# Attention and two feed-forward layers on one core: loads cut to the rows with data, a spread by ScalarE, all block inverses on GpSimd, other PSUM banks in the prologue

## The reference

```python
for t in range(S):
    y[:, :, t] = einsum('bhd,bhde->bhe', rt, state)
    Sa = einsum('bhde,bhe->bhd', state, at)
    state = state * wt[:, :, None, :] - einsum('bhd,bhe->bhde', Sa, bt) + einsum('bhd,bhe->bhde', vt, kt)
h = x @ w_in;   solu = h * softmax(h);   x = (layernorm(solu) * g_ln) @ w_out
h = x @ w2_in;  x = (max(h, 0) + alpha * min(h, 0)) @ w2_out
```

## Time and profile before

| | before |
|---|---|
| median of 3 runs | 1088.87 us |
| profiled execution, its own time | 1090.63 us |
| its span | 1088.6 us |
| mean granted clock of TensorE | 0.945 of full |
| busy: PE, DVE, ACT, POOL | 955.0, 642.5, 406.1, 224.3 us |
| last store of attention issued | at about 489 us |

### The profile page before, as it was taken

How to read it: one execution, slowest core, us unless ns; L and a number is a source line. 1 busy time by engine, 2 the same in 40 slices (tenths; PEclk the granted TensorE clock), 3 DMA queues, 4 the chain that set the end, 5 groups by cost and what they waited for, 6 DMA issues and landing times.

```text
span 1088.6 us, 32820 instructions
## 1 busy us (share of the span) xinstructions
PE 955.0 (88%) x14112; PEld 903.2 (83%) x14112; DVE 642.5 (59%) x1120; ACT 406.1 (37%) x842; POOL 224.3 (21%) x442
## 2 busy tenths in 40 slices
PE   3377889788978888885899999999999999999998
PEld 2366778677867877874899999999999999999987
DVE  6864666475756764357465564746546474664644
ACT  2112333242423342325444353534435363443533
POOL 4362463355336434200000000000000000000000
PEclk9588999898999999896999999999999999999999
DMA  7527455655665564316200000000000000000000
GB/s 259 103 78 187 119 153 132 169 139 166 167 142 161 158 170 102 90 43 182 62 2 25 11 15 25 2 24 0 24 12 12 24 0 24 0 24 12 2 13 13
DMA packets 145925, 82.91 MB, mean 76 GB/s; under 512 B 119824, under 2 KB 129168, under 8 KB 145808
## 3 DMA queue, kind: packets, MB, share of 16 engines
q1 hardware_dynamic: 145808, 81.17, 27.4%
HBM read 61.49 MB, written 19.66 MB: 75 GB/s over the span
## 4 chain that ended last, share of the span: by engine, by line
PE 61%; issue 14%; POOL 10%; DVE 6%; SPq 6%; DMA 2%; ACT 1%; DVEq 0%; ACTq 0%; POOLq 0%
PE acc L916 6%; PE acc L918 5%; PE acc L917 5%; PE bank L916 5%; PE bank L918 5%; PE bank L917 5%; POOL s_x L695 4%; PE mid L916 4%; PE mid L918 4%; PE mid L917 4%; POOL s_t L693 4%; SPq L202 4%; PE px L292 2%; PE mid L969 2%; PE mid L970 2%
## 5 line engine op out<-in xcount | busy, mean ns | idle before, releaser
L1250 DVE SCALAR_TENSOR_TENSOR stage<-mid,slope 128x512 f32<-128x512 f32 x96 | 66.4, 692 | 110.0 <-ACT slope L1092 110.0
L1146 POOL TENSOR_TENSOR stats<-stats,consts 128x1 f32<-128x1 f32 x24 | 13.2, 549 | 571.5 <-DVE stats L1228 571.5
L916 PE MATMUL acc<-wo_h,act_h 128*128 128x320 f32 x384 | 122.5, 319 | 7.2 <-DVE act_l L1160 6.4
L918 PE MATMUL acc<-wo_l,act_h 128*128 128x320 f32 x384 | 119.3, 311 | 0.0
L917 PE MATMUL acc<-wo_h,act_l 128*128 128x320 f32 x384 | 119.2, 311 | 0.0
L1088 ACT ACTIVATE stage<-mid 128x512 f32<-128x512 f32 x96 | 57.3, 597 | 162.3 <-PE mid L970 162.3
L267 PE MATMUL pa<-al,wkb 128*64 128x128 f32 x768 | 67.7, 335 | 50.8 <-issue 28.7
L916 PE MATMUL mid<-zT_h,w_h 128*128 128x256 f32 x384 | 108.9, 284 | 0.7 <-DVE zT_s L1160 0.7
L918 PE MATMUL mid<-zT_l,w_h 128*128 128x256 f32 x384 | 108.9, 284 | 0.0
L917 PE MATMUL mid<-zT_h,w_l 128*128 128x256 f32 x384 | 108.9, 284 | 0.0
L267 PEld LDWEIGHTS pa<-al,wkb 128*64 128x64 f32 x768 | 55.9, 172 | 53.8 <-issue 30.3
(11 more groups left out here) (122 smaller groups left out, 2396.0 us busy)
## 6 DMA issues: line engine op xcount, KB each, us to landing
wkb<-wkb_features_first SPq DMA_DIRECT2D x24, 776.0 KB, 6.2
al<-a_features_first SPq DMA_DIRECT2D x24, 512.0 KB, 5.0
rvu<-rv_features_first SPq DMA_DIRECT2D x48, 160.0 KB
l_scr<-lb SPq DMA_DIRECT2D x24, 256.0 KB, 4.5
x_scr<-x SPq DMA_DIRECT2D x24, 256.0 KB, 4.2
sv<-v_time_first SPq DMA_DIRECT2D x48, 80.0 KB, 5.5
out<-y_sb SPq DMA_DIRECT2D x12, 320.0 KB, 2.3
d_scr<-s_x SPq DMA_DIRECT2D x12, 256.0 KB, 2.3
```

The source lines that it names most:

```text
L916: pe.matmul(o, left[0], right[0], start=start, stop=False)
L918: return pe.matmul(o, left[0], right[1], start=False, stop=stop)
L1250: dve.scalar_tensor_tensor(out=act_f[q % 2][:], in0=mid[q % 2][:], scalar=0.0, in1=slope[q % 2][:], op0=ALU.max, op1=ALU.add).then_inc(act ...
```

## The change

- From the fourth chunk (wkb) and the seventh (a) on, a load brings only the 40 rows with data of each half, and of a only the block that is not zero. One DMA of 128 rows becomes two of 40. The rows that are left out still hold what the first use of the buffer brought.
- For a this is not enough, since `mask_ka` overwrites the zeros in al. So from chunk 6 on ScalarE copies the two scaled blocks into `a_bd`, a tile whose other blocks GpSimd has set to zero once, and the scores read that.
- GpSimd runs `scale_a(n + 6)` ahead of `solve` in odd steps. It also inverts pair 0, ahead of the prologue's memsets, and `solve_first` goes.
- SyncE's even step has `d_read` ahead of the loads of wkb and v. In the prologue `l_write(1)` and `l_read(1)` stand ahead of `d_write(0)`, and ScalarE issues half of the eight DMAs of `d_read(0)`.
- In the prologue the scores go to the banks pa and pq in turn, and the transposes of k and b to px and pr, so that one chunk need not wait for the other.
- The first x tile goes into a staging buffer, which moves two weight loads from step 14 to the end of step 15; a separate x buffer and a constant's tile go.

```diff
+    a_bd = sb("a_bd", [P, 2, NH, T])
...
+    def score_banks(m):
+
+        return pq if m in (1, 3) else pa
...
         def load_wkb(m):
             wait(sp, kbn_done, 2 * (m - 2))
-            sp.dma_start(wkb[m % 3][:], wkb_in[m]).then_inc(wkb_loaded[m % 3], 16)
+            if m < 3:
+                sp.dma_start(wkb[m][:], wkb_in[m]).then_inc(wkb_loaded[m], 16)
+            else:
+                for h in range(2):
+                    sp.dma_start(wkb[m % 3][ER[h]], wkb_in[m, ER[h]]).then_inc(wkb_loaded[m % 3], 16)
 
         def load_a(m):
             wait(sp, rhs_done, m - 5)
-            sp.dma_start(al[m % 6][:].rearrange("p a h t -> p (a h t)"), a_in[m]).then_inc(a_loaded[m % 6], 16)
+            if m < 6:
+                sp.dma_start(al[m][:].rearrange("p a h t -> p (a h t)"), a_in[m]).then_inc(a_loaded[m], 16)
+            else:
+                for h in range(2):
+                    sp.dma_start(al[m % 6][ER[h], h].rearrange("p h t -> p (h t)"),
+                                 a_in[m, ER[h], h * NH * T:(h + 1) * NH * T]).then_inc(a_loaded[m % 6], 16)
...
         def step(n):
...
             if n + 6 < NG:
                 load_a(n + 6)
+            if n % 2 == 0 and n + 2 < NG:
+                d_read((n + 2) // 2)
             if n + 7 < NG:
                 load_wkb(n + 7)
             if n + 2 < NG:
                 load_v(n + 2)
-            if n % 2 == 0 and n + 2 < NG:
-                d_read((n + 2) // 2)
...
         def scores(m, piece):
-            pe.wait_ge(a_ready, 2 * m + 2)
-            wait(pe, kbn_ready, 2 * m - 1 + piece)
+            if m < 6:
+                pe.wait_ge(a_ready, 2 * m + 2)
+            else:
+                pe.wait_ge(a_bd_ready, 2 * (m - 6) + 2)
+            if m < AHEAD:
+                wait(pe, l_ready, 4 * (m - 2) + 4)
+                wait(pe, ka_ready, 4 * (m - 2) + 4)
+            else:
+                pe.wait_ge(kbn_ready, 2 * m - 1 + piece)
...
+        def spread_a(m):
+
+            if m == 6:
+                act.wait_ge(a_bd_set, 1)
+            act.wait_ge(a_ready, 2 * m + 2)
+            wait(act, l_done, 2 * m)
+            for half in range(2):
+                act.copy(a_bd[ER[half], half], al[m % 6][ER[half], half]).then_inc(a_bd_ready, 1)
...
             scale_a(2)
             scale_a(3)
+            pool.wait_ge(masks_loaded, 16)
+            solve(0)
             for z in rvu[1:]:
                 pool.memset(z[:], 0.0).then_inc(rvu_set, 1)
             pool.wait_ge(rvu_set, 3)
             scale_a(4)
+            pool.memset(dd[1][:], 0.0).then_inc(dd_set, 1)
+            pool.wait_ge(dd_set, 2)
+            solve(1)
...
         def step(n):
+            if n + 6 < NG:
+                scale_a(n + 6)
             if n % 2 == 1 and n + 3 < NG:
                 solve((n + 3) // 2)
-            if n + 6 < NG:
-                scale_a(n + 6)
```

More of the change, by code:

```diff
@@ L185, in d_write, with d_read @@
         def d_write(p):
[L186 to L189, removed]
+            sp.wait_ge(solve_step, (p + 1) * SOLVE)
             sp.dma_start(d_scr[p].rearrange("k l x -> l k x"),
                          s_x[:].rearrange("p k s t -> p k (s t)")).then_inc(d_out[p % 2], 16)
-        def d_read(p):
+        def d_read(p, blocks=range(2 * NB)):
             if p < 2:
@@ L197, in d_read @@
             sp.wait_ge(d_out[p % 2], use(p, 2, 16))
[L198 to L203, removed]
+            for b in blocks:
+                sp.dma_start(*d_block(p, b)).then_inc(d_back[p % 2], 16)
         def save_y(m):
@@ L217, in prologue @@
                 load_a(m)
+            l_write(0)
             load_wkb(3)
-            l_write(0)
+            l_read(0)
             load_wkb(4)
-            l_read(0)
             for m in range(2):
@@ L224, in prologue @@
                 load_rv(m)
+            l_write(1)
+            load_wkb(5)
+            l_read(1)
             d_write(0)
[L226 to L229, removed]
+            d_read(0, range(0, 2 * NB, 2))
             load_wkb(6)
@@ L273, in turn_kb @@
             for piece in range(2):
-                pe.wait_ge(l_ready, 4 * m + 2 + 2 * piece)
-                pe.wait_ge(ka_ready, 4 * m + 2 + 2 * piece)
-                for h in range(piece * 4, piece * 4 + 4):
-                    ins = pe.transpose(pa[:, h * P:(h + 1) * P], kbT[m % 3][:, h].rearrange("p a b -> p (a b)"), ident)
+                if m < AHEAD - 1:
+                    wait(pe, kbn_ready, 2 * m - 1 + piece)
+                    bank = [px, pr][piece]
+                else:
+                    pe.wait_ge(l_ready, 4 * m + 2 + 2 * piece)
+                    pe.wait_ge(ka_ready, 4 * m + 2 + 2 * piece)
+                    bank = pa[:, piece * 512:piece * 512 + 512]
+                for i in range(4):
+                    ins = pe.transpose(bank[:, i * P:(i + 1) * P],
+                                       kbT[m % 3][:, piece * 4 + i].rearrange("p a b -> p (a b)"), ident)
                 ins.then_inc(kbn_done, 1)
@@ L380, in prologue @@
                 scores(m, 1)
-                turn_kb(m)
-            for stage in range(4):
+                if m < AHEAD - 1:
+                    turn_kb(m)
+            horner(0, 0)
+            turn_kb(AHEAD - 1)
+            for stage in range(1, 4):
                 horner(0, stage)
@@ L637, in prologue @@
                     take_kbn(m)
+            d_read(0, range(1, 2 * NB, 2))
             take_rhs(0)
@@ L646, in step @@
             take_uT(n)
+            if front and n + AHEAD >= 6:
+                spread_a(n + AHEAD)
             if 0 < n < NG - 1:
@@ L772, in feed_forward @@
     stage2 = sb("stage2", [P, 1024])
-    x_in = [early["x_in"], sb("x_in1", [P, KT, 2 * P])]
+    x_in = [sb(f"x_in{i}", [P, KT, 2 * P]) for i in range(2)]
+    first_x = stage[1][:, 0:KT * 2 * P].rearrange("p (k t) -> p k t", k=KT)
     soft = [sb(f"soft{i}", [P, FF1]) for i in range(2)]
@@ L1139, in gpsimd @@
     def gpsimd(pool):
-        pool.memset(consts[:], -0.5).then_inc(chain, 1)
+        pool.memset(consts, -0.5).then_inc(chain, 1)
         pool.wait_ge(chain, 1)
```

140 lines of the change are left out of this document (67 added, 73 removed).

## The result

| | before | after |
|---|---|---|
| median of 4 runs each, on one chip | 1090.36 us (1087.03 to 1094.14) | 1125.9 us (1117.3 to 1128.5) |
| profiled execution, its span | 1090.63, 1088.6 | 1117.3, 1115.5 |
| mean granted clock of TensorE | 0.945 | 0.928 |
| busy PE, DVE, ACT, POOL, us | 955.0, 642.5, 406.1, 224.3 | 947.0, 636.5, 428.9, 244.0 |

The change makes the kernel 3.1% slower: the ratio is 1.0307, 95% interval 1.025 to 1.0364. The forecast was 1089 us with a range up to 1102. The profiled execution of after is the fastest of its four runs, so what is read from it is at the low end of what the change costs: its span shows 26.9 us of the 35.5 by which the medians differ.

What follows compares the result with a forecast made beforehand. Bound: until 390 us the loop for each pair of chunks through SyncE and GpSimd, not TensorE. Shift of the end: -3 + 8 x 0.5 + 1.2 - 2.2 = 0, so 1089 us, range 1074 to 1102.

Steps and rivals of the forecast that it cites:

- The bounds given for l_read to the inverse: Odd step, start of GpSimd's inverse: between 6.2 us behind l_read (+2.5) and 9.2 (+5.5).
- the 7.4: Odd step: with scaling ahead, the inverse starts 7.4 us behind l_read instead of 3.76, +3.6 a round.
- The inverse itself: GpSimd's inverse in each round: escapes part of VectorE's front, 14.2 us instead of 15.96, -1.8.
- The upper bound that I gave, 0: GpSimd's inverse in each round: its change was put between -3.6 and 0.
- I leave at 4.68: SyncE's wait for l_write in each round: unchanged at 4.68 us, between 0 and +1.0.
- third rival: SyncE's loop: l_write waits behind wkb, +1.0 a round more than forecast, +8, 1097 us; chance 0.07.
- the rounds begin 3 us earlier: Prologue: inverse of pair 2 comes at 100.5 to 101 us against 103.43, though chunk 0 starts 4 us later.
- +0.5 a round: Loop per pair: -1.4, +3.6 and -1.8 sum to +0.4, called +0.5, eight times: +4.
- The load of a lands with l_read: Odd step: +2.5, inverse escapes most of the front (-2.6), round 1.5 shorter, 1073 us; chance 0.32.
- second rival: Loop: a lands no sooner, scaling collides with VectorE's front, +2.3 a round, 1103 us; chance 0.18.
- The fourth: SyncE's loop: d_read's issue is not shortened from 7.55 us, +3.5 a round, 1115 us; chance 0.03.
- The rule of forty rows: Loads of wkb: 40 rows use ten engines, so 485 KB weigh like 776 KB on sixteen; loads no shorter.

Runs made afterwards that it cites:

- e1: Changed kernel with GpSimd's old order, inverting first and scaling a behind it: 1092.1 us, ratio to before 1.0029.
- e6: Kernel before, with d_read put ahead of the loads of wkb and v: 1090.5 us, ratio to before 1.0002.
- e2: Changed kernel with SyncE's old order, the loads of wkb and v ahead of d_read: 1108.6 us, ratio to before 1.0179.
- e12: Changed kernel with the even step's loads of wkb and v moved behind l_write: 1113.0 us, ratio to before 1.0202.
- e15: Changed kernel unaltered, measured again beside the last experiments: 1120.2 us, ratio to before 1.0276.
- e7: Kernel before, with GpSimd scaling a ahead of the inverse: 1130.2 us, ratio to before 1.0342.
- e4: Changed kernel with wkb loaded whole (one DMA of 128 rows), still behind d_read: 1112.1 us, ratio to before 1.0171.
- e10: Changed kernel with 48 rows of each half instead of 40 in the loads of wkb and a: 1130.2 us, ratio to before 1.0368.
- e3: Changed kernel with both old orders, SyncE's and GpSimd's, put back: 1078.0 us, ratio to before 0.9878.
- e11: Changed kernel with both old orders, SyncE's and GpSimd's, and wkb loaded whole: 1085.8 us, ratio to before 0.9949.
- e5: Kernel before, with wkb from chunk 3 on loaded as two DMAs of 40 rows: 1092.8 us, ratio to before 1.0003.
- e9: Changed kernel with loads of a, wkb and v moved behind l_read, only one a left in the even step, behind l_write: 1069.0 us, ratio to before 0.981.
- e8: Changed kernel with the odd step's load of a issued a step earlier, right behind l_write: 1100.05 us, ratio to before 1.0075.
- e13: Changed kernel with no bulk load between d_write and l_read except a behind l_write, and wkb loaded whole: 1074.1 us, ratio to before 0.9826.
- e14: Kernel before, with bulk loads moved behind l_read, one a behind l_write, and scaling ahead of the inverse: 1080.5 us, ratio to before 0.9898.

## Why the prediction was wrong

**Right.** d_read's issue at 4.03 in the round shown and 4.28 in the mean (forecast 4.03); l_write's end at 11.99 (11.65); the inverse 7.59 behind l_read in the mean, its scaling released by a's load (7.4, +3.6; measured +3.4); TensorE's step 3.7 us earlier in the round (forecast 4), its wait for scaled a gone and its idle time in one piece ahead of the even chunk's horner. VectorE's scan came late, as forecast (12.97 in the round shown; 13.8), and held nothing there: TensorE ran from 289.07 to 301.39 without a gap. ScalarE's spread does not show as a cost in any column. The bounds given for l_read to the inverse (+2.5 to +5.5) held for the mean.

**Right in part by luck.** No round had the 7.4. Four had 6.3 to 6.6, with a in 3.8 to 4.1 us behind l_read and not 4.9, and three had 8.3 to 9.7. The forecast knew neither group; its value lies between them.

**Failed: "The inverse itself", -1.8 a round; measured +0.5.** The step supposed that an inverse that starts later, while TensorE's step starts earlier, leaves part of a front of VectorE to the scaling. Both shifts came, and the inverse still did not get shorter: 15.73 instead of 14.2, and 15.0 to 15.2 in five of the seven rounds. Two things were missed. TensorE works at the lower clock when it comes back from its idle stretch (7.04 us instead of 4.77 to its second product), so the front comes only 1.4 us earlier in the round than before (23.50 against 24.91) and lies wholly behind the inverse's start at 23.38. And the next front is no longer held back by TensorE's wait for scaled a. It begins 37.6 to 38.7 us behind d_write in five of the seven rounds, inside the inverse, where before it began 8.3 to 8.9 behind the next d_write, outside; so even in the fourth and the sixth round, where the first front began over 4 us ahead of the inverse and only its last scan reached into it, it took 15.23. I had moved one front and not the one behind it. The row that I took the step from was high as well, 15.96 against a mean of 15.23 before, which makes 0.7 of the miss; the rest, 1.5, is the front that did not escape. The upper bound that I gave, 0, was itself too low. In e1, with the old order of GpSimd, the inverse takes 15.39. This error is 2.3 us a round.

**Failed: the wait for l_write "I leave at 4.68"; measured 5.97 in the mean against 4.39, +1.6 a round.** The one row of before with a wkb load right ahead had shown 5.67, and the 3 us of issuing that I let speak for 0 do not help, since issuing is not landing: at 287 us the DMA engines still move 39 GB/s, and the wkb issued at 285.98 releases VectorE's scan only at 292.57, behind l_write's issue. e6 shows +1.16 for this order alone, e2 takes 1.3 away and e12 0.9. This was the third rival's mechanism, to which I gave 0.07 and +1.0.

**Failed: "the rounds begin 3 us earlier"; measured 0.8.** l_write(1) and l_read(1) came as forecast (57.87 against 58.3), but d_write(0) stood behind it for 2.57 us of issue and d_read(0) followed at 63.28, not 61.4, so that chunk 0's horner began at 68.76 instead of 66, 6.6 later than before. The forecast gave 0.4 us to a d_write whose queue had just taken rows of wkb:

```profile
53.55 3.48 SPq L168 DMA_DIRECT2D wkb<-wkb_features_first  x2
57.87 0.39 SPq L205 DMA_DIRECT2D s_in<-l_scr  x1
58.30 2.57 SPq L210 DMA_DIRECT2D d_scr<-s_x  x1
...
63.28 2.23 SPq L219 DMA_DIRECT2D dd<-d_scr  x4
```

**The sum.** Forecast +0.5 a round, measured +3.8: 2.3 of the gap is the inverse and 1.6 the wait, and the smaller terms take back 0.6. Times eight that is 27 us, with the prologue 29, of the 29.9 at chunk 22's horner; the feed-forward part, which the forecast left as it was, gives 4.3 back. The loop was the right place to look and its length the right unit; the error came in with each round.

**The rivals.** "The load of a lands with l_read" (0.32) came true in its first half in four of the seven rounds, +2.5 to +3.0 over the same rounds of before; its second half, the inverse that escapes the front, did not, so its time did not come either. The second rival, scaled a on the loop, with a late and the scaling beside a front, describes the other three; in the mean its size was that of the forecast's term and not its 5.5, and the 7.6 us that were to mark it are just what was measured (7.59, and 7.99 in e15). The fourth, that d_read is not shortened, is excluded by 4.28. What came in the mean was the forecast's own +3.6 together with the third rival, and the gain that was to pay for it did not come. The two edits that I added up with opposite signs, e6 and e7, are worth 0 and +3.4% alone.

**The rule of forty rows.** The wait for l_write was no shorter with less to load: 5.97 us with 485 KB in loads of 40 rows, 5.44 with 776 KB of 128 rows (e4). The Trainium skill (DMA: Bandwidth & Descriptors, the section on why a DMA increments its semaphore by 16) says that a DMA takes the largest number of engines up to 16 that divides its rows, so ten for 40 rows, and sixteen for 48. By that rule e10 should have had a wait under after's. It had 6.04 against 5.97 to 6.08, and 9.73 from l_read to the inverse. So the direction of the rule agrees with e4, and e10 speaks against it as the cause here; what makes rows of wkb worse ahead of l_write than the whole is open. So is whether rows of wkb give anything beside the old orders (e3 is 0.7% under e11, with intervals that touch); on the kernel before they give nothing (e5).

## What to carry to other kernels

Before putting a step ahead of the chain's own, ask what that step waits for: here 2.4 us of scaling brought a load that is issued behind the chain's own read, and it cost 3.4 us a round in the mean. In an in-order queue, a shorter issue is not a gain until the next transfer on the chain lands; put the bulk loads where the chain has nothing in flight and the engine waits for arithmetic (e9), not between its transfers. When terms of opposite sign are added, shift every engine's schedule by the same delays, the next occurrence of the other engine's work too, before claiming that an overlap goes away. And look at every round, not at one: a mean can be right although no round is.

## What the runs showed that was not expected

- Two loads of 40 rows of wkb (485 KB) ahead of l_write left it 5.97 us to wait (5.97 to 6.52 in the profiles of after, e1, e8 and e15), one of 128 rows (776 KB) 5.44 (e4 alone); with nothing but reads and small loads between, it waits 4.8 to 5.1 (e9, e12, e13, e14), and with wkb ahead of the reads 4.4 to 4.8 (before, e2, e3, e11).
- An issue shows the backlog of its queue: the eight reads of 32 KB each took 4.03 us to issue behind 160 KB of a, 7.58 in the mean behind 512 and 776 KB, and 5.8 behind the rows of both; a write that takes 0.39 us to issue in the loop took 2.57 behind rows of wkb in the prologue.
- After the last of those reads is issued, the DMA engines go on for 2 us at 39 to 62 GB/s, and move 333 GB/s in the window from 289 us on.
- VectorE's scan or product of two tensors goes with a longer GpSimd operation beside it: small ones of the inverse 1.05 to 1.3 us instead of 0.25, the masking of 128 x 256 1.86 instead of 0.85, the scaling of a 3.3 to 3.7 instead of 2.4. VectorE's own scan took 1.72 instead of 1.26.
- TensorE, back from 11.05 us of idleness, worked for the first 5 us at a granted clock of 0.50: its horner took 1.97 us instead of 1.15.
